# The load of the first two value chunks moves from SP's queue to GpSimd's queue, behind a wait

## What is computed

```
state = alpha[t][:, None] * state + outer(k[t], v[t]);  y[t] = q[t] @ state     # per head: 8 heads of 48
h = gelu(x @ w_in);  u, v = split(h);  v_n = layernorm(v) * g_ln                 # x is y by token, 384 wide
x1 = x + (u * (w_sg @ v_n + b_sg)) @ w_out
u = x1 + real(fft(fft(x1, axis=1), axis=2))
out = u + relu(layernorm(u) @ w_ch1) @ w_ch2
```

## Time and profile before

| what | us |
|---|---|
| median of 3 executions | 768.94 |
| lowest and highest | 763.87, 770.72 |
| the profiled execution | 763.87 |
| its span in the profile | 762.1 |
| mean granted clock of PE over the span | 0.991 of full |

### The profile page before, as it was taken

One profiled execution on the slowest core, in us unless ns is written; L12 is line 12 of the kernel. 1 busy time (PEld: TensorE's weight loads), 2 busy tenths in 40 slices (PEclk: granted clock), 3 DMA queues, 4 the chain that ended last, 5 costly groups with the idle time before them and its releaser, 6 DMA issues.

```text
span 762.1 us, 12002 instructions
## 1 busy us (share of the span) xinstructions
PE 741.9 (97%) x4860; PEld 718.7 (94%) x4860; DVE 459.4 (60%) x872; ACT 195.0 (26%) x366; POOL 76.5 (10%) x122
## 2 busy tenths in 40 slices
PE   8899999999999999999987899999999999999997
PEld 7789999899998999989987899999999999999997
DVE  7999777896758967566757835445353635432221
ACT  1345111432113311134222521213211332122111
POOL 1022000120002100051024022001210010000000
PEclk9999999999999999999996999999999999999999
DMA  9632314313122131081245023001120020000000
GB/s 281 193 89 89 90 52 116 88 49 88 53 79 79 47 94 48 32 231 42 70 148 188 1 63 97 9 33 63 37 68 1 31 62 31 0 31 1 1 32 31
DMA packets 21000, 54.04 MB, mean 71 GB/s; under 512 B 2356, under 2 KB 14776, under 8 KB 20952
## 3 DMA queue, kind: packets, MB, share of 16 engines
q1 hardware_dynamic: 18104, 44.53, 19.6%
q0 software_dynamic: 2704, 8.71, 3.8%
q10 hardware_dynamic: 144, 0.13, 0.1%
HBM read 43.90 MB, written 9.46 MB: 70 GB/s over the span
## 4 chain that ended last, share of the span: by engine, by line
PE 91%; DVE 5%; DMA 2%; issue 1%; ACT 1%; POOL 0%; DVEq 0%; SPq 0%
PE bank L1078 75%; PE bank L1136 5%; PE bank L1109 3%; PE bank L1132 2%; PE bank L1124 2%; PE bank L1275 1%; PE bank L1099 1%; DMA u_new<-x_scratch,mirrored_rows 1%; DVE u_kept L1034 1%; PE bank L1167 1%; DMA decay_k_q<-in_akq 1%; PE bank L1084 0%; DVE fwd_b L835 0%; DVE fwd L835 0%; DVE rev_b L823 0%
## 5 line engine op out<-in xcount | busy, mean ns | idle before, releaser
L1078 PE MATMUL bank<-ut_hi,w_c_parts 128*128 128x384 f32 x576 | 163.7, 340 | 1.3 <-DVE ut_lo L1011 1.3
L1025 DVE SCALAR_TENSOR_TENSOR hidden_lo<-bank,hidden_hi 128x384 fp32r<-128x384 f32 x96 | 53.3, 555 | 127.5 <-ACT hidden_hi L753 126.4
L1078 PEld LDWEIGHTS bank<-ut_hi,w_c_parts 128*128 128x128 f32 x576 | 105.7, 188 | 1.6 <-issue 1.5
L753 ACT ACTIVATE hidden_hi<-bank 128x384 fp32r<-128x384 f32 x96 | 47.3, 492 | 200.4 <-PE bank L1078 200.3
L1078 PE MATMUL bank<-w_c_hi,hidden_hi 128*128 128x384 f32 x288 | 96.5, 335 | 0.7 <-DVE u_kept L1034 0.7
L1078 PE MATMUL bank<-ut_lo,w_c_parts 128*128 128x384 f32 x288 | 96.6, 335 | 0.0
L1078 PE MATMUL bank<-w_c_hi,hidden_lo 128*128 128x384 f32 x288 | 96.3, 335 | 0.0
L1078 PE MATMUL bank<-w_c_lo,hidden_hi 128*128 128x384 f32 x288 | 96.2, 334 | 0.0
L1078 PE MATMUL bank<-w_sg_hi,vn_hi 128*128 128x384 f32 x192 | 66.2, 345 | 0.7 <-ACT u_gelu L689 0.7
L1078 PE MATMUL bank<-w_sg_hi,vn_lo 128*128 128x384 f32 x192 | 64.2, 334 | 0.0
L1078 PE MATMUL bank<-w_sg_lo,vn_hi 128*128 128x384 f32 x192 | 64.2, 334 | 0.0
(11 more groups left out here) (177 smaller groups left out, 1478.6 us busy)
## 6 DMA issues: line engine op xcount, KB each, us to landing
decay_k_q<-in_akq SPq DMA_DIRECT2D x19, 673.8 KB, 5.3
x_scratch<-x_half SPq DMA_DIRECT2D x8, 579.0 KB, 3.9
out_tiles<-u_kept SPq DMA_DIRECT2D x24, 192.0 KB, 2.0
values<-in_v SPq DMA_DIRECT2D x18, 192.0 KB, 5.2
x_quarters<-x_scratch SPq DMA_DIRECT2D x16, 168.9 KB, 5.6
raw_first_a<-in_w_first SPq DMA_DIRECT2D x3, 768.0 KB, 4.2
raw_first_b<-in_w_first SPq DMA_DIRECT2D x3, 768.0 KB, 5.3
raw_weights_b<-in_w_second SPq DMA_DIRECT2D x3, 768.0 KB, 4.3
```

The costliest lines, as they stand in the source:

```text
L753: nc.scalar.activation(hid[0][:, i % 4, :], HB[i % 2][:, 0:HS], ACT.Relu).then_inc(hhi_done, 1)
L1025: nc.vector.scalar_tensor_tensor(out=hid[1][:, i % 4, :], in0=HB[i % 2][:, 0:HS], scalar=0.0, in1=f32(hid[0][:, i % 4, :]), op0=ALU.max, o ...
L1078: ins = nc.tensor.matmul(dst, a, c, start=start and n == 0, stop=stop and n == len(passes) - 1)
```

## The change

The load of the values of chunks 0 and 1 leaves SP's list. It is issued by POOL instead, ahead of POOL's other load, and only once the keys and queries of chunk 0 have landed. The other loads of SP keep their order and are issued one place earlier.

```diff
@@ block.sync
-            load_first(1)
-            sp.dma_start(val_first[:, 0:2, :], v_in[0:2].rearrange("c p n -> p c n")).then_inc(val_first_in[0], 16)
-            load_first(2)
-            load_first(3)
+            for c in range(1, 4):
+                load_first(c)
             load_piece(sp, 0)
             load_piece(sp, 1)
             load_first(4)
@@ block.gpsimd
             nc.gpsimd.memset(eps_c[:], EPS)
             nc.gpsimd.memset(mhalf[:], -0.5).then_inc(memset_done, 1)
+            pool.wait_ge(akq_in[0], 16)
+            pool.dma_start(val_first[:, 0:2, :], v_in[0:2].rearrange("c p n -> p c n")).then_inc(val_first_in[0], 16)
             pool.wait_ge(akq_in[2], 16)
             pool.dma_start(val_first[:, 2:NT, :], v_in[2:NT].rearrange("c p n -> p c n")).then_inc(
                 val_first_in[1], 16)
```

## The result

The changed kernel takes 770.66 us in the median of 20 executions (768.99 to 781.08), against 766.44 us for the kernel before (lowest 763.65, 20 executions, one of which took 2573.63 us; without it the median is 765.76). The ratio is 1.0058, with a 95% interval from 1.0038 to 1.0079: slower by 0.6%, inside the 1% that the prediction called no change, on the side that it named. The profiled execution took 769.57 us with a span of 767.7 us, 5.7 and 5.6 us more than before.

The account below looks back on a forecast made before the run. PE bounds most of the kernel, but DVE the early stretch using the moved load. SP's 0, 3.0 us of lateness and 2.2 us of clock gave 5.2 us on 768.94: 774.1 us, range 766 to 780.

Parts of the forecast that it names:

- What bounds the stretch: From 6.18 to 31.54 us DVE bounds; a hole in its order there goes to the end in full.
- SP's side: On SP's queue chunk 2 could land 1.2 us sooner, into time it already has: gain none.
- POOL's issue and the landing: POOL issues the values at about 6.4 us; beside SP's full queue they take 9.0 us and land at 15.4.
- The cost of the landing: PE's out 0 starts 3.7 us late, 0.7 us is free, so DVE's chunk 1 mask product is 3.0 us late.
- The clock: PE stands 4.0 us before out 0; its clock falls, adding 2.2 us to out 0 and scores 1, bounds 0 to 4.2.
- The sum: Whole kernel: 0 + 3.0 + 2.2 = 5.2 us, added to a median of 768.94 us for 774.1 us, 0.7% more.
- A: Rival: the values land in time, at 11.2 us, so nothing changes, 768.9 us; chance 0.13.
- B: Rival: values late before out 0, but PE's clock holds, 771.9 us; chance 0.17.
- C: Rival: POOL's load waits behind SP's queued loads and takes 12.8 us; clearly slower, 777.9 us, up to 779.9; chance 0.18.

Follow-up runs that it names:

- experiment 4: The changed kernel with SP holding back chunks 2 and 3 and the weight pieces until the values have landed: 771.97 us, ratio 1.0048 to the kernel before.
- Experiment 1: The changed kernel with POOL's load of the values issued without its wait for chunk 0's keys and queries: 768.70 us, ratio 1.0018 to the kernel before.
- experiment 7: The kernel of experiment 5, with the values issued on SP behind chunk 2 instead of ahead of it: 765.38 us, ratio 0.9994 to the kernel before.
- experiment 6: The changed kernel with 21 idle products ahead of out 0 and 7 ahead of the scores of chunk 3: 768.33 us, ratio 1.0023 to the kernel before.
- experiment 3: The changed kernel with 21 instead of 5 idle products ahead of out 0, keeping PE busy while it waits: 772.05 us, ratio 1.0057 to the kernel before.
- experiment 2: The kernel before with the values still loaded on SP without a wait, but behind chunks 2 and 3: 771.34 us, ratio 1.0064.
- experiment 5: The kernel before with 7 idle products in PE's stop ahead of the scores of chunk 3, run twice: 764.59 and 766.43 us, ratios 0.9985 and 0.9984.

## Why the prediction was right

**What bounds the stretch: right.** DVE's order carried the delay undiminished to the first product, and it was still there at 392 us. SP's side gave nothing: chunk 2 did land sooner (2.10 + 8.3 = 10.4 us) and DVE did not use it.

**POOL's issue and the landing: right.** Issue at 6.00 us against 6.4, 8.8 us against 9.0, landing at 14.8 against 15.4. Most of the 0.6 us between comes from outside: chunk 0's keys and queries landed at 5.70 us, 0.39 us sooner than in the profile of before, and shifted all that follows. That load takes 4.5 to 4.9 us in the profiles of all the kernels here, without a pattern, so this belongs to the execution. The reason given, that SP's full queue is what makes POOL's load slow, is confirmed by experiment 4: 3.7 us without it. Experiment 1 shows it from the other side: issued 4.7 us sooner it still took 9.7 us. The estimate by the rule of the Trainium skill, "DMA: Bandwidth & Descriptors", section "Anatomy of one DMA — SWDGE (gpsimd) path", was 2.9 us; the 3.7 us of experiment 4 come near it, the 8.8 us do not.

**The cost of the landing: right.** Out 0 was 3.13 us late (3.7 forecast) and 0.7 us of it was free, which leaves 2.4 us (3.0 forecast). The room of 0.7 us was shown by experiment 7, the price by experiment 6.

**The clock: right in kind, too small in size.** The clock fell in the wait, and PE restarted at 0.50. The term was put at 2.2 us, from a ratio of 1.52 between idle products at either clock. The stretch took 7.92 instead of 4.23 us, a ratio of 1.87, so the term is 3.7 us, inside the bounds 0 to 4.2. The step that failed is the choice of the row, for two reasons. The time of one matmul in a group depends on how many there are (42 idle matmuls took 4.96 us in experiment 3, 118 ns each, where 10 took 138 ns each), and the two groups had different counts. And the row is the end of a group of 20 that starts at 406.21 us, cut by the view's window: it runs to 410.47 us, and the clock was at 0.50 only to 409.75 us and at 0.78 from there on, so a part of it was not at half speed. Like with like, the eight idle matmuls ahead of out 1 took 2.07 us in the changed kernel and 1.16 before, a ratio of 1.78. The sum of the three, 3.13 - 0.69 + 3.69 = 6.13 us, is the 6.16 us by which DVE's mask product was late. The rule of the Trainium skill named for it, "TensorE: Matmul & The Clock Gate", section "HAM oscillation — how this bites in real kernels", that a wait for a transfer makes PE restart at half clock, agrees with this: the clock was at 0.50 when the load ended.

**The sum: near, with some luck.** It said 5.2 us. The profiles show 5.7, the fastest executions 5.3 (768.99 against 763.65), the medians 4.2 (4.9 without the execution of 2573.63 us). At the first product, which the sum is about, it was 6.2; a lateness put 0.6 us too high and a clock put 1.5 us too low partly cancel. That the median moved less than the profile has a likely reason, which is not shown: the kernel before pays for falls of the clock of its own in many executions. Its mean clock is 0.980 to 0.987 in most of those over 767 us, against 0.989 to 0.991 in those near 763, but only one execution of it was profiled, one of 763.87 us. Where such falls can lie, other kernels show: behind the stop ahead of the scores of chunk 3 (experiments 1, 3 and 4) and at 103 to 123 us (experiments 2, 3, 5 and 6). The changed kernel has nearly lost that stop, since PE comes there late, and has no execution below 768.9 us. The median that the sum was added to, 768.94 us of three executions, was high; 20 gave 766.44. The predicted 774.1 lies 3.4 us above the measured 770.66: 2.5 us of that is the base and 1.0 the sum.

**The rivals.** A (in time) and B (the clock holds) did not occur in either profile of the changed kernel. Above 774.1 us, 1% over the 766.44 of before, were four of the 26 executions, but C's mechanism is not what the runs point to: both profiles of the changed kernel have the landing at 8.8 us, and three of the four executions have a mean clock of 0.967, which in experiment 2's profile meant a clock at 0.50 for longer. Of the rows that the prediction named for the changed profile two came later than said, both by the clock term: DVE's mask product of chunk 1 at 22.80 us (19 to 22 forecast) and the first product at 37.84 us (36 to 37). The others were as said.

## What to carry to other kernels

A load that is needed early is priced by when it lands beside what is queued with it, not by its own size: here 384 KB took 3.7 us beside an almost empty queue and 8.8 us beside a full one. A wait for it costs its length beyond the room that the next engine has, and once more what the stop does to PE's clock; here that was 2.4 us and 3.7 us. When idle work fills one stop, look for the next stop before expecting the time, and look along the whole profile: a clock that falls 70 us further on can hide an effect of 3 us.

## What the runs showed that was not expected

The executions of the kernel before fall into two groups, 38 of 87 from 762.6 to 765.2 us and 45 from 767.0 to 773.4, from the same code and on the same chips; filling its stop of 1.75 us left 7 of 24 over 767 us. The fall behind that stop came in experiments 1, 3 and 4 and not in the profile of before, though the stop is 1.75 or 1.76 us in all of them. Nor is a long stop needed: the falls between 103 and 123 us come where the largest stop of PE is 0.66 us, in five profiles of twelve. The length of a stop alone does not say whether the clock falls.
